# Reordered first transfers and a later rounding of U and V in a retention and gating kernel

## What is computed

```python
# retention: 2 batches x 8 heads, 768 positions, head size 64
state = gamma * state + k_t (outer) v_t          # for each t
y_t   = scale * q_t @ state                      # x = y with the heads side by side: [2, 768, 512]
# mixing and a first MLP
h  = (x^T @ U @ V)^T                             # U: 768x32, V: 32x768, over positions
u  = x + h
x2 = u + relu(u @ w_ch1) @ w_ch2                 # 512 -> 2048 -> 512
# spatial gating
a  = relu(x2 @ w_in); uu, v = halves of a        # 512 -> 1024
v_s = w_spatial @ normalise(v) + b_spatial
out = (uu * v_s) @ w_out
```

## Time and profile before

| | us |
|---|---|
| median of 3 runs | 487.36 |
| lowest and highest of them | 486.97, 489.19 |
| the profiled execution | 487.95 |
| its span, from the first to the last instruction | 486.2 |
| TensorE busy in it | 472.6 (97%) |
| VectorE, ScalarE, GpSimd busy | 200.9, 169.3, 101.6 |
| start of slot 1, 2, 3 (first scores of items 1, 2, 3) | 15.43, 23.95, 31.27 |

### The profile page before, as it was taken

How to read it: one execution, slowest core, us unless ns; L and a number is a source line. 1 busy time by engine, 2 the same in 40 slices (tenths; PEclk the granted TensorE clock), 3 DMA queues, 4 the chain that set the end, 5 groups by cost and what they waited for, 6 DMA issues and landing times.

```text
span 486.2 us, 7182 instructions
## 1 busy us (share of the span) xinstructions
PE 472.6 (97%) x2736; PEld 405.6 (83%) x2736; DVE 200.9 (41%) x339; ACT 169.3 (35%) x301; POOL 101.6 (21%) x87
## 2 busy tenths in 40 slices
PE   4999989999999999999999999999999989999997
PEld 3788878888888888888888888888888879999997
DVE  3888886322326533222223531223222873521530
ACT  1444355323336424323233413233232741222212
POOL 1554521232223211222222111222221050000000
PEclk9999999999999999999999999999999999999999
DMA  7999932600000000000000005000002000011003
GB/s 287 414 319 319 330 138 90 256 0 0 0 1 1 0 1 0 0 0 0 0 1 2 0 1 226 0 0 0 0 0 88 0 1 1 1 65 66 0 1 129
DMA packets 8150, 33.30 MB, mean 68 GB/s; under 512 B 832, under 2 KB 2496, under 8 KB 5824
## 3 DMA queue, kind: packets, MB, share of 16 engines
q1 hardware_dynamic: 8128, 32.98, 18.3%
HBM read 29.84 MB, written 3.15 MB: 68 GB/s over the span
## 4 chain that ended last, share of the span: by engine, by line
PE 89%; DVE 4%; DMA 4%; SPq 1%; ACT 1%; issue 1%; POOLq 0%; POOL 0%; DVEq 0%
PE bank L1022 10%; PE bank L937 9%; PE bank L939 9%; PE bank L938 9%; PE bank L927 9%; PE bank L929 9%; PE bank L928 9%; PE bank L1037 7%; PE bank L951 2%; PE bank L956 2%; PE bank L952 2%; DMA ident<-eye 2%; PE bank L817 2%; DMA w1raw<-w 2%; PE bank L983 1%; PE bank L982 1%
## 5 line engine op out<-in xcount | busy, mean ns | idle before, releaser
L338 POOL TENSOR_TENSOR w2l<-w2raw,w2h 128x512 fp32r<-128x512 f32 x48 | 63.9, 1332 | 214.2 <-ACT w2h L437 214.2
L670 DVE SCALAR_TENSOR_TENSOR hl<-bank,hh 128x512 fp32r<-128x512 f32 x48 | 33.2, 691 | 167.8 <-ACT hh L443 167.8
L927 PE MATMUL bank<-uth,w1h 128*128 128x512 f32 x192 | 75.0, 391 | 0.9 <-DVE utl L660 0.7
L929 PE MATMUL bank<-uth,w1l 128*128 128x512 f32 x192 | 74.7, 389 | 0.0
L928 PE MATMUL bank<-utl,w1h 128*128 128x512 f32 x192 | 74.7, 389 | 0.0
L937 PE MATMUL bank<-hh,w2h 128*128 128x512 f32 x192 | 74.7, 389 | 0.0
L938 PE MATMUL bank<-hl,w2h 128*128 128x512 f32 x192 | 74.7, 389 | 0.0
L939 PE MATMUL bank<-hh,w2l 128*128 128x512 f32 x192 | 74.7, 389 | 0.0
L443 ACT ACTIVATE hh<-bank 128x512 fp32r<-128x512 f32 x48 | 28.7, 598 | 89.1 <-PE bank L929 89.1
L437 ACT ACTIVATE w2h<-w2raw 128x512 fp32r (+1 forms) x48 | 30.2, 630 | 66.3 <-PE bank L939 66.3
L927 PEld LDWEIGHTS bank<-uth,w1h 128*128 128x128 f32 x192 | 36.1, 188 | 8.9 <-DVE utl L660 1.1
(11 more groups left out here) (86 smaller groups left out, 682.9 us busy)
## 6 DMA issues: line engine op xcount, KB each, us to landing
att<-attn SPq DMA_DIRECT2D x7, 1152.0 KB, 8.5
w1raw<-w SPq DMA_DIRECT2D x4, 1024.0 KB, 7.9
w2raw<-w SPq DMA_DIRECT2D x4, 1024.0 KB, 8.4
att<-attn SPq DMA_DIRECT2D x10, 384.0 KB, 5.8
out_T<-stage SPq DMA_DIRECT2D x7, 384.0 KB, 2.3
tab<-decay SPq DMA_DIRECT2D x8, 258.0 KB, 5.0
winraw<-w_in SPq DMA_DIRECT2D x1, 2048.0 KB, 11.4
wsp_raw<-w_sp SPq DMA_DIRECT2D x1, 1920.0 KB, 7.3
```

What stands on the lines that cost most here:

```text
L338: nc.gpsimd.tensor_tensor(w2l[k][:, :], w2raw[:, f, :], raw(w2h[k])[:, :], ALU.subtract).then_inc(w2_lo, 1)
L670: nc.vector.scalar_tensor_tensor(out=hl[k][:, :], in0=hid_ps[k][:, :], scalar=0.0, in1=raw(hh[k])[:, :], op0=ALU.max, op1=ALU.subtract).th ...
L927: mm(hid_ps[k][:, :], w1h[k][:, s], uth[t % 2][:, c, :], start=(c == 0), stop=False)
L929: m = mm(hid_ps[k][:, :], w1l[k][:, s], uth[t % 2][:, c, :], start=False, stop=(c == CT - 1))
```

## The change

The first item's transfers are issued by SP and ACT together: q and k of chunks 1 and 2, and the table, by ACT at the start of its program, the other four by SP. SP then waits for `kv_group` (k and v of chunks 0 to 2 of item 0) before it issues q and k of item 1, and for `qk_loaded[0]` (the last transfer of item 0) before item 1's table and v, the identity (with a semaphore of its own now), U and V; then it waits for U before it issues the first quarter of w1, and everything that stands behind that in SP's program stands behind this wait too. ACT rounds U in slot 1 between `sc_copy(1, 1)` and `p_round(0)`, and V behind `p_round(0)`; DVE takes U's rest between `mask_a(1, 1)` and `states(1)`, and V's between `p_rest(0)` and `decay_q(2)`. `turn` waits for the identity alone.

```diff
--- before.py
+++ after.py
@@ -151,6 +151,7 @@
         tab_loaded = [sem(f"tab_loaded{k}") for k in range(2)]
         vraw_loaded = sem("vraw_loaded")
         cst_loaded = sem("cst_loaded")
+        eye_loaded = sem("eye_loaded")
         w1_loaded = sem("w1_loaded")
         w2a_loaded = sem("w2a_loaded")
         w2b_loaded = sem("w2b_loaded")
@@ -254,17 +255,18 @@
 
             first = attn[0, :, :].rearrange("p (a s) -> p a s", a=4)
             sp.dma_start(att[0][:, 0:2, 0:P], first[:, 0:2, 0:P]).then_inc(qk_first, 16)
-            sp.dma_start(att[0][:, 0:2, P:HS], first[:, 0:2, P:HS]).then_inc(qk_group, 16)
-            load_tab(0, 0)
             sp.dma_start(att[0][:, 2:4, 0:HS], first[:, 2:4, 0:HS]).then_inc(kv_group, 16)
             sp.dma_start(att[0][:, 2:4, HS:S], first[:, 2:4, HS:S]).then_inc(v_loaded[0], 16)
             sp.dma_start(att[0][:, 0:2, HS:S], first[:, 0:2, HS:S]).then_inc(qk_loaded[0], 16)
+            sp.wait_ge(kv_group, 16)
             load_qk(1, 1)
+            sp.wait_ge(qk_loaded[0], 16)
             load_tab(0, 1)
+            load_v(1, 1)
+            sp.dma_start(ident[:, :], eye).then_inc(eye_loaded, 16)
+            sp.dma_start(urep[:, :, :], u_rep).then_inc(cst_loaded, 16)
             sp.dma_start(vraw[:, :], v_rep).then_inc(vraw_loaded, 16)
-            load_v(1, 1)
-            sp.dma_start(urep[:, :, :], u_rep).then_inc(cst_loaded, 16)
-            sp.dma_start(ident[:, :], eye).then_inc(cst_loaded, 16)
+            sp.wait_ge(cst_loaded, 16)
             sp.dma_start(w1raw[:, 0:4, :], w1[:, 0:4, :]).then_inc(w1_loaded, 16)
             with sp.Fori(0, NI // 2 - 1) as j:
                 for k in range(2):
@@ -372,6 +374,10 @@
 
         @block.scalar
         def _(act):
+            first = attn[0, :, :].rearrange("p (a s) -> p a s", a=4)
+            act.dma_start(att[0][:, 0:2, P:HS], first[:, 0:2, P:HS]).then_inc(qk_group, 16)
+            act.dma_start(tab[0][:, :], decay[0, :, :]).then_inc(tab_loaded[0], 16)
+
             def sc_copy(i, g):
                 act.wait_ge(sc_done, 2 * i + g + 1)
                 if not (isinstance(i, int) and i < 1):
@@ -398,18 +404,20 @@
                 xn_copy(i - 1, 0)
                 xn_copy(i - 1, 1)
                 sc_copy(i, 1)
+                if i == 1:
+                    act.wait_ge(cst_loaded, 16)
+                    nc.scalar.activation(ust[:, :, :], urep[:, :, :], ACT.Copy).then_inc(ust_hi, 1)
                 p_round(i - 1)
+                if i == 1:
+                    act.wait_ge(vraw_loaded, 16)
+                    nc.scalar.activation(vst[:, :], vraw[:, :], ACT.Copy).then_inc(v_hi, 1)
                 xt_copy(i, 0, k)
                 xt_copy(i, 1, k)
 
             sc_copy(0, 0)
             sc_copy(0, 1)
             xt_copy(0, 0, 0)
-            act.wait_ge(vraw_loaded, 16)
-            nc.scalar.activation(vst[:, :], vraw[:, :], ACT.Copy).then_inc(v_hi, 1)
             xt_copy(0, 1, 0)
-            act.wait_ge(cst_loaded, 32)
-            nc.scalar.activation(ust[:, :, :], urep[:, :, :], ACT.Copy).then_inc(ust_hi, 1)
             for i in range(1, NI - 1):
                 slot(i)
 
@@ -625,9 +633,19 @@
                 xn_rest(i - 1, 0)
                 xn_rest(i - 1, 1)
                 mask_a(i, 1, k, pair)
+                if i == 1:
+                    dve.wait_ge(cst_loaded, 16)
+                    dve.wait_ge(ust_hi, 1)
+                    nc.vector.tensor_tensor(ust[:, :, 3 * R:P], urep[:, :, 3 * R:P], raw(ust)[:, :, 3 * R:P],
+                                            ALU.subtract).then_inc(ust_lo, 1)
                 states(i, 0, NC - 2, k)
                 states(i, NC - 2, NC - 1, k)
                 p_rest(i - 1)
+                if i == 1:
+                    dve.wait_ge(vraw_loaded, 16)
+                    dve.wait_ge(v_hi, 1)
+                    nc.vector.tensor_tensor(vst[R:2 * R, :], vraw[R:2 * R, :], raw(vst)[R:2 * R, :],
+                                            ALU.subtract).then_inc(v_lo, 1)
                 decay_q(i + 1, 1 - k, (i + 1) // 2)
                 u_add(i - 1, (i - 1) // 2, 1 - k)
 
@@ -643,14 +661,6 @@
             mask_a(0, 1, 0, 0)
             decay_q(1, 1, 0)
 
-            dve.wait_ge(vraw_loaded, 16)
-            dve.wait_ge(v_hi, 1)
-            nc.vector.tensor_tensor(vst[R:2 * R, :], vraw[R:2 * R, :], raw(vst)[R:2 * R, :],
-                                    ALU.subtract).then_inc(v_lo, 1)
-            dve.wait_ge(cst_loaded, 32)
-            dve.wait_ge(ust_hi, 1)
-            nc.vector.tensor_tensor(ust[:, :, 3 * R:P], urep[:, :, 3 * R:P], raw(ust)[:, :, 3 * R:P],
-                                    ALU.subtract).then_inc(ust_lo, 1)
             for i in range(1, NI - 1):
                 slot(i)
 
@@ -868,7 +878,7 @@
             def turn(i, g, k):
 
                 pe.wait_ge(xt_done, 2 * i + g + 1)
-                pe.wait_ge(cst_loaded, 32)
+                pe.wait_ge(eye_loaded, 16)
                 if g and i:
                     pe.wait_ge(u_done, 2 * i - 1)
                 for c in range(G):
```

## The result

| | before | changed |
|---|---|---|
| median of 8 executions each | 487.64 us | 490.62 us |
| lowest, highest | 486.97, 489.19 | 488.57, 492.03 |
| ratio, 95% interval | | 1.0057, 1.0042 to 1.0072 |
| profiled execution, its span | 487.95, 486.2 | 491.97, 490.2 |
| start of slot 1, 2, 3 in it | 15.43, 23.95, 31.27 | 13.79, 24.55, 35.30 |

A forecast was written before the change was run, and what follows sets the result against it. TensorE's own work bounds settled slots, so only waits before them can change. Terms -0.6 - 1.2 + 1.2 + 0.5 = -0.1 us take the profiled 487.95 to 487.85, forecast median 487.3, range 485.8 to 489.2.

The forecast's parts named there:

- Part 1: Item 0's transfers: issuing two on ACT's queue lands the last one sooner, -0.6 us (bounds 0 and -1.8); slot 1 at 14.83.
- Part 2: Start of slot 1: the identity lands sooner and U's and V's rounding no longer precede the scores' copies, -1.2 us.
- Part 3: Slot 1: U's rounding on ACT and its rest on VectorE delay the down matmuls with no cover, +1.2 us.
- Part 4: Slot 2: V's rest costs 0.1; item 2's table, issued behind SP's wait for U, delays qd, +0.5 us (0.2 to 1.2).
- Rival 2: Queue runs dry behind the wait for U, item 2 late: slot 3 at 33.95, +2.7 us, 490.0; chance 0.15.
- Rival 1: Item 0 is faster alone, without item 1's transfers: slot 1 at 13.6, -1.6 us, median 485.8; chance 0.27.
- Rival 3: The second queue brings nothing, item 0's landings stay as before: +0.5 us, 487.9; chance 0.15.

The follow-up runs named there:

- experiment 2: Kernel before with only two of item 0's transfers (q and k of chunks 1 and 2, the table) moved to ACT's queue; median 486.59 us, ratio 0.9981.
- experiment 9: Kernel before with second queue, w1's first quarter behind item 2, U and identity loaded before V, U rounded between item 0's output copies, V in slot 1; 486.76 us.
- experiment 1: Changed kernel without SP's wait for U ahead of w1's first quarter; median 488.42 us, ratio 1.0018 to the kernel before.
- experiment 5: Changed kernel with 14 filler matmuls of the identity ahead of slot 2's scores; median 490.21 us, ratio 1.0048 to the kernel before.
- experiment 6: Changed kernel with 7 filler matmuls of the identity ahead of slot 2's scores; median 489.16 us, ratio 1.0026 to the kernel before.
- experiment 4: Kernel before with only the rounding of U and V moved into slot 1, transfers as before; median 488.83 us, ratio 1.0025.
- experiment 3: Kernel before with only SP's two waits holding back item 1's and later transfers, all on SP's queue, no wait for U; median 488.47 us, ratio 1.0022.

## Why the prediction was wrong

- **Part 1** (-0.6) was right in its sign and too small. Item 0 gained 1.64 in the profile, but part of that is luck of the execution: in the nine profiles with the second queue qd is released at 8.13 to 8.56 (9.88 and 10.03 in the two kernels with the first transfers as before), and slot 1 starts at 13.79 to 14.72, 14.37 in the middle (15.43 and 15.71). Some 1.2 us is the better figure, and the changed kernel's 13.79 is the earliest of the nine. The estimate of 0.2 MB more by 3 us fails: the changed kernel moved no more in the first 3 us (55 GB/s), and the last piece landed 1.4 us sooner all the same. From 3 to 8 us experiment 2 moves 389 GB/s, where the kernel before moves 333 and the one with only the holding back 319. Why that is more isn't settled. The rule of the Trainium skill that I set beside it (DMA: Bandwidth & Descriptors, section "Issuing engines are not separate DMA queues": a second issuing engine saves the issue time only) isn't fully borne out: the last transfer left SP 1.0 us sooner, and even the smallest gain between those profiles is 1.3 us.
- **Part 2** (-1.2): the 1.23 us of slot 1 are U's roundings and the identity, as experiment 9 shows, where both are out of the way (1.68). In the changed kernel's profile it was 2.19, because the held-back table of item 1 released qd only at 13.26, beside kd, for 2.19 us, and the mask of slot 1 stood behind it. I had not priced holding item 1's table back. It showed since slot 1 started so early there: in experiments 1, 5 and 6, with the same order but slot 1 at 14.44 to 14.72, its second scores come 1.67 to 1.68 behind, as forecast.
- **Part 3** (+1.2) held to 0.04 us: 1.24 in the changed kernel and in experiment 4.
- **Part 4** (+0.5) is the step that failed: the lateness of item 2's transfers behind SP's wait for U. The place and the order were right, the size was not. I had q and k of item 2 landing between 22.0 and 23.0 and the table at 23.1; they landed at 24.5 and 25.2. U landed at 15.3 instead of 14.6 (the two gains that the text names, 0.3 MB and 0.6 us, would even give 13.7), SP took 0.9 us from w1's issue to item 2's, and 362 GB/s were moved from 17.5 on instead of 409. From 15.5 to 24.5 some 2.86 MB were moved, 0.6 more than the 2.23 that I had counted: V's end and transfers issued behind item 2's share the time. The wait for q and k cost 1.68 us, and the table behind them 1.43 us in slot 2. V's rest alone ended at 22.17, as harmless as forecast, because here the table, and so kd, came later still.
- **What the sum had no term for** is the clock. I counted a wait as its own length; this one was followed by some 6.6 us at half the granted clock, 2.0 us in the profile and 1.5 in the median when filler took its place.
- **These two are the whole miss in the profile.** The second scores of slot 2 hang on the table alone: 25.25 for qd, then 2.41 for qd, u and the mask, as I had added it up. The table 2.1 us late and the clock 2.0 make 4.1, the distance from my slot 3 at 31.2 to the 35.30 measured. What parts 1 to 3 had right or wrong no longer counts behind such a wait.
- **Rival 2** was the right one, with its mechanism (the queue runs dry behind the wait for U, item 2 late). I gave it 0.15, and of that only a third to beyond 0.5%, although its bounds rested on rates that the first 8 us did show. That its price, 490.0, is near the 490.6 measured is partly luck: it had the table at 25.9 and no fall of the clock. With the table at 25.2 its own sum gives slot 3 at 33.3, 2.0 us late; the clock made up the rest. **Rival 1** had the early slot 1 (before 14.2), but by another mechanism than its own: holding item 1 back gives item 0 0.7 us on one queue (experiment 3) and nothing on top of the second one. **Rival 3** was wrong by experiment 2.

What stays open: the mean price of V's rest (between the 0.1 that I gave it and the 1.4 of experiment 4's profile), and how often the clock falls in the changed kernel: three of its eight executions have the full mean clock and take 488.57 to 490.21, two with 0.997 take 490.4 and 490.8, and the three with 0.993 take 491.6 to 492.0. Why it falls in some and not in others no trace shows.

## What to carry to other kernels

A wait put ahead of a transfer holds everything behind it in that queue's program: list what stands there and when each is needed, before asking what the wait protects. Small work that is moved into a full slot is priced by what runs beside it: an operation of VectorE with two SBUF inputs that starts just behind one of GpSimd takes the rest of that one on top of its own time. And where a change may put a new wait of TensorE into a full stretch, as the 1.62 us here, a term for the clock belongs in the sum: it cost as much again as the wait. A gap alone needn't do it; the 1.24 us ahead of down left the clock at 1.00 in the profiles of experiments 1 and 4.

## What the runs showed of the hardware that I had not expected

- Gaps of 1.24 us (ahead of 18.89) and 1.62 us (ahead of 24.55) were followed by a granted clock of 0.50 from some 25.5 to 32.1, in a program in which TensorE is 97% busy before the change; at it 12 matmuls took 1.65 us instead of 0.94. With filler in the second gap the clock stayed at 1.00.
- At the start of every run the same 12 matmuls take 1.65 us too, though the profile shows a granted clock of 1.00 there. When they become fast differs between executions that are alike until then: slot 1 started at 13.79 in the changed kernel, and at 14.66 in the run with 14 filler matmuls, whose qd also started at 8.42.
- Two transfers moved from SP's to ACT's queue brought the last of six forward by 1.5 us, 0.5 more than its earlier issue, with 389 GB/s moved from 3 to 8 us in place of 333.
- An operation of VectorE with two SBUF inputs that starts just behind one of GpSimd takes 2.13 to 2.19 us in place of 0.95 (V's rest) and 2.15 in place of 0.83 (qd); started 0.08 us ahead, it is GpSimd's kd that takes 2.16 in place of 1.55.
